# Clustered attention with two feed-forward layers: where the softmax division is done, which engine makes the one-hot comparisons, and the order of TensorE's work in a tile

## The reference

```
q_assign = argmax(normalised q . normalised centroids)      # 16 clusters
k_assign = argmax(normalised k . normalised centroids)
scores   = where(q_assign == k_assign, q k^T / 8, -1e9)
attn     = exp(scores - rowmax);  attn = attn / (rowsum + 1e-9)
out      = attn @ v
x = out as 1536 x 512
h = x @ w_in (512 x 2048);  g = P(h) / (Q(h) + 1e-6);  x = g @ w_out
h = x @ w_in2;              g = h - tanh(h);           out = g @ w_out2
```

## Time and profile before

| | |
|---|---|
| median of three runs | 822.11 us (821.48 to 824.07) |
| the profiled execution | 823.63 us, with a span of 821.8 us from the first to the last instruction |
| mean granted TensorE clock | 0.983 of full speed |
| PE busy | 791.9 us, 96% of the span |
| PEld busy | 680.3 us, 83% |
| DVE busy | 526.7 us, 64% |
| ACT busy | 501.5 us, 61% |
| POOL busy | 353.0 us, 43% |

### The profile page before, as it was taken

One profiled execution on the slowest core, in us unless ns is written; L12 is line 12 of the kernel. 1 busy time (PEld: TensorE's weight loads), 2 busy tenths in 40 slices (PEclk: granted clock), 3 DMA queues, 4 the chain that ended last, 5 costly groups with the idle time before them and its releaser, 6 DMA issues.

```text
span 821.8 us, 11654 instructions
## 1 busy us (share of the span) xinstructions
PE 791.9 (96%) x4066; PEld 680.3 (83%) x4066; DVE 526.7 (64%) x910; ACT 501.5 (61%) x954; POOL 353.0 (43%) x377
## 2 busy tenths in 40 slices
PE   5899999999999899999999999999999999999998
PEld 5789998989898787888788888888888888888886
DVE  4599889898988879999977787995311211111111
ACT  3578788888888877878776777777422222222222
POOL 5467787877877723213222222226622222222222
PEclk7699999999999999999999999999999999999999
DMA  4723323332330205200000011115100100001001
GB/s 129 188 72 76 85 73 83 85 77 72 83 74 19 68 11 154 77 0 1 1 0 1 1 51 52 52 52 170 35 1 1 51 1 1 0 9 44 1 0 52
DMA packets 39082, 41.17 MB, mean 50 GB/s; under 512 B 4720, under 2 KB 30320, under 8 KB 39024
## 3 DMA queue, kind: packets, MB, share of 16 engines
q1 hardware_dynamic: 39024, 40.42, 17.5%
HBM read 26.25 MB, written 3.15 MB: 36 GB/s over the span
## 4 chain that ended last, share of the span: by engine, by line
PE 55%; POOL 20%; DVE 13%; issue 6%; ACT 3%; SPq 2%; DMA 1%; POOLq 0%; DVEq 0%; ACTq 0%
PE y_ps L1060 27%; PE h_ps L1039 25%; POOL probs L407 9%; DVE f_bc L841 2%; DVE f_t L860 2%; DVE w_lo L815 2%; DVE f_bc L858 2%; POOL nq L416 2%; DVE f_a L854 2%; POOL v L433 1%; POOL nk L424 1%; POOL hot L441 1%; POOL x_lo L452 1%; DVE f_t L846 1%; POOL hot L442 1%
## 5 line engine op out<-in xcount | busy, mean ns | idle before, releaser
L498 POOL TENSOR_TENSOR g_lo<-f_t,g_hi 128x512 fp32r<-128x512 f32 x96 | 125.1, 1303 | 377.7 <-ACT g_hi L594 377.7
L897 DVE TENSOR_TENSOR f_t<-h_ps,f_a 128x512 f32<-128x512 f32 x48 | 33.2, 691 | 203.4 <-ACT f_a L673 203.4
L1039 PE MATMUL h_ps<-x_hi,w_hi 128*128 128x512 f32 x384 | 149.5, 389 | 1.3 <-DVE w_lo L815 1.3
L1039 PE MATMUL h_ps<-x_lo,w_hi 128*128 128x512 f32 x384 | 149.5, 389 | 0.0
L1039 PE MATMUL h_ps<-x_hi,w_lo 128*128 128x512 f32 x384 | 149.4, 389 | 0.0
L594 ACT ACTIVATE g_hi<-f_t 128x512 fp32r<-128x512 f32 x96 | 60.8, 633 | 138.8 <-PE y_ps L1060 123.4
L407 POOL TENSOR_SCALAR probs<-probs,rinv 128x768 f32<-128x768 f32 x96 | 86.3, 911 | 69.2 <-DVE rinv L782 65.9
L557 ACT ACTIVATE pt_hi<-pt_ps 128x384 fp32r<-128x384 f32 x192 | 85.3, 492 | 48.3 <-PE pt_ps L979 47.1
L788 DVE TENSOR_TENSOR pt_lo<-pt_ps,pt_hi 128x384 fp32r<-128x384 f32 x192 | 98.5, 547 | 13.8 <-ACT pt_hi L557 13.1
L775 DVE TENSOR_REDUCE nmax<-s_ps 128x1 f32<-128x768 f32 x96 | 91.0, 948 | 7.4 <-PE s_ps L966 6.5
L979 PE MATMUL pt_ps<-ident,probs 128*128 128x128 f32 x576 | 85.1, 283 | 6.7 <-POOL probs L407 5.6
(11 more groups left out here) (122 smaller groups left out, 1571.7 us busy)
## 6 DMA issues: line engine op xcount, KB each, us to landing
w_raw<-in_moe_w_in_dram SPq DMA_DIRECT2D x32, 256.0 KB, 2.9
w_raw<-in_moe_w_out_dram SPq DMA_DIRECT2D x32, 256.0 KB, 3.7
ka<-qk_b SPq DMA_DIRECT2D x32, 192.0 KB, 3.0
raw_q<-in_q_dram SPq DMA_DIRECT2D x16, 192.0 KB, 2.6
raw_k<-in_k_dram SPq DMA_DIRECT2D x16, 192.0 KB, 2.9
raw_v<-in_v_dram SPq DMA_DIRECT2D x16, 192.0 KB, 3.1
qk_b<-qa SPq DMA_DIRECT2D x16, 192.0 KB, 2.7
out_dram<-f_bc SPq DMA_DIRECT2D x12, 256.0 KB, 2.1
```

The source lines that it names most:

```text
L498: pool.tensor_tensor(g_lo[n % 2][:, :], f_t[n % 2][:, :], g_hi[n % 2][:, :].bitcast(F32), ALU.subtract).then_inc(g_lo_done, 1)
L897: dve.tensor_tensor(f_t[n % 2][:, :], h_ps[n % 4][:, :], f_a[n % 2][:, :], ALU.subtract).then_inc(g_done, 1)
L1039: last = pe.matmul(h_ps[n % 4][:, :], w[f][:, ws], x[:, cols], start=(kt == 0 and i == 0), stop=(kt == KT - 1 and i == 2))
```

## The change

The softmax division leaves the probabilities. They are transposed and multiplied with v undivided; the division is made on the finished `xf` (128 rows: two heads of 64 dimensions; 384 columns: positions). There the reciprocal belongs to a column, so the reciprocals of a half head (128 partitions x 3 columns) go by DMA to a row of 384 numbers in DRAM (`rows_out`) and back, broadcast to the 64 partitions of that head (`rows_in`); POOL multiplies (`normalise`). `row_inverse` runs once in three turns on three columns. The comparisons of `finish_hot` move from DVE to POOL in another form (subtract, then max and add, or max and multiply); the first two heads keep them on DVE (`finish_first`). On POOL `rank_hot` goes ahead of `split_k`, the two `x_low` of a pair are set apart, on ACT `copy_x` is one turn later, and on PE `score_tile` comes ahead of the units.

```diff
 # tensors
+        z_rows = nc.dram_tensor("z_rows", [HALVES, HALF], F32, kind="Internal").ap()
+        rz = [sb(attn_mem, f"rz{i}", [P, HALF]) for i in range(2)]
-        POOL_CHUNK_AT = {79: 0, 83: 1, 85: 2, 91: 3}
+        POOL_CHUNK_AT = {80: 0, 83: 1, 86: 2, 92: 3}
 # SP
+            def rows_out(hh):
+                sp.wait_ge(rinv_done, hh + 1)
+                sp.dma_start(z_rows[hh, :].rearrange("(t p) -> p t", p=P),
+                             rinv[:, HT * hh % 12:HT * hh % 12 + HT],
+                             allow_slow_non_contiguous=True).then_inc(z_out, 16)
+            def rows_in(hh):
+                s, half = divmod(hh, 2)
+                sp.wait_ge(z_out, 16 * (hh + 1))
+                if s >= 2:
+                    sp.wait_ge(norm_done, 2 * (s // 2 - 1) + half + 1)
+                sp.dma_start(rz[half][D * (s % 2):D * (s % 2) + D, :],
+                             z_rows[hh, :].partition_broadcast(D)).then_inc(rz_in[half], 16)
             for k in range(-1, TILES):
+                if k >= 0 and k % HT == 1:
+                    rows_out(k // HT)
+                if k > 0 and k % HT == 0:
+                    rows_in(k // HT - 1)
 ...
+            rows_in(HALVES - 1)
 # POOL
-            def scale_probs(m):
-                pool.wait_ge(rinv_done, m + 1)
-                hi_of(probs[m % PROBS][:, :], probs[m % PROBS][:, :], rinv[:, m % 12:m % 12 + 1]).then_inc(probs_scaled, 1)
+            def finish_hot(g):
+                pool.wait_ge(top2_done, g - FIRST + 1)
+                pool.wait_ge(prep_done, prepared(g - 1, HOT))
+                link(pool.tensor_tensor(hot_nat[:, :, :].rearrange("p a (t c) -> p (a t) c", c=C), hot[:, :, :],
+                                        top2[:, :].unsqueeze(2).broadcast_to([P, 2 * T, C]), ALU.subtract))
+                pool.tensor_scalar(hot_nat[:, 0, :], hot_nat[:, 0, :], -1.0, 1.0, ALU.max, ALU.add).then_inc(hot_done, 1)
+                pool.tensor_scalar(hot_nat[:, 1, :], hot_nat[:, 1, :], -1.0, BIG, ALU.max, ALU.mult).then_inc(hot_done, 1)
+            def normalise(pair, half):
+                pool.wait_ge(rz_in[half], 32 * (pair + 1))
+                pool.wait_ge(xf_done, 4 * pair + 2 + half + 1)
+                pool.tensor_tensor(xf[half][:, :], xf[half][:, :], rz[half][:, :], ALU.mult).then_inc(norm_done, 1)
-            for m in range(2):
-                scale_probs(m)
             for k in range(TILES):
                 if r == 0 and 3 <= (k + 18) // T < HEADS:
                     split_q((k + 18) // T)
-                if r == 1 and 3 <= (k + 17) // T < HEADS:
-                    split_k((k + 17) // T)
-                if r == 2 and 2 <= (k + 10) // T < HEADS:
-                    rank_hot((k + 10) // T)
+                if r == 1 and 2 <= (k + 11) // T < HEADS:
+                    rank_hot((k + 11) // T)
+                if r == 2 and 3 <= (k + 16) // T < HEADS:
+                    split_k((k + 16) // T)
                 if r == 3 and 1 <= (k + 3) // T < HEADS:
                     split_v((k + 3) // T)
-                if r == 5:
-                    s = (k - 11) // T
-                    if s >= 1 and s % 2 == 1:
-                        x_low(s // 2, 0)
-                        x_low(s // 2, 1)
+                if r == 4 and 2 <= (k + 8) // T < HEADS:
+                    finish_hot((k + 8) // T)
+                if r in (1, 4) and k // T >= 2 and k // T % 2 == 0:
+                    normalise(k // T // 2 - 1, r // HT)
+                if r == 5 and k // T >= 2 and k // T % 2 == 0:
+                    x_low(k // T // 2 - 1, 0)
+                if r == 0 and k // T >= 3 and k // T % 2 == 1:
+                    x_low(k // T // 2 - 1, 1)
-                if k % 2 == 0 and k + 2 < TILES:
-                    scale_probs(k + 2)
-                    scale_probs(k + 3)
             split_weights(PRELOAD)
+            normalise(LAST_PAIR, 0)
             g_low(0)
+            normalise(LAST_PAIR, 1)
             g_low(1)
 # ACT
             def copy_x(pair, half):
-                act.wait_ge(xf_done, 4 * pair + 2 + half + 1)
+                act.wait_ge(norm_done, 2 * pair + half + 1)
-                if s >= 1 and s % 2 == 1 and r in (1, 4):
-                    copy_x(s // 2, (0 if r == 1 else 1))
+                if s >= 1 and s % 2 == 1 and r in (2, 5):
+                    copy_x(s // 2, r // HT)
 # DVE
-            def row_inverse(m, count):
-                cols = slice(m % 12, m % 12 + count)
-                dve.wait_ge(exp_done, m + count)
+            def row_inverse(hh):
+                cols = slice(HT * hh % 12, HT * hh % 12 + HT)
+                dve.wait_ge(exp_done, HT * hh + HT)
+                if hh >= 4:
+                    dve.wait_ge(z_out, 16 * (hh - 3))
                 link(dve.tensor_scalar(rsum_e[:, cols], rsum[:, cols], 1e-9, None, ALU.add))
-                dve.reciprocal(rinv[:, cols], rsum_e[:, cols]).then_inc(rinv_done, count)
+                dve.reciprocal(rinv[:, cols], rsum_e[:, cols]).then_inc(rinv_done, 1)
-                if r == 3 and 2 <= (k + 9) // T < HEADS:
-                    finish_hot((k + 9) // T)
-                if k % 2 == 0 and k + 2 < TILES:
-                    row_inverse(k + 2, 2)
+                if k % HT == 0:
+                    row_inverse(k // HT)
 # PE
             def transpose_probs(k):
-                pe.wait_ge(probs_scaled, k + 1)
+                pe.wait_ge(exp_done, k + 1)
             for k in range(TILES):
                 transpose_probs(k)
+                if k + LOOK < TILES:
+                    score_tile(k + LOOK)
                 for g, u in units_at[k]:
                     if u != SIM:
                         unit(g, u)
-                if k + LOOK < TILES:
-                    score_tile(k + LOOK)
                 if k >= HT:
                     values(k)
```

More of the change, by code:

```diff
@@ L179, in clustered_attention_then_two_ffns @@
         max_done, rinv_done, pt_lo_done = sem("max_done"), sem("rinv_done"), sem("pt_lo_done")
-        sim_read, top_done, xf_done = sem("sim_read"), sem("top_done"), sem("xf_done")
-        k_lo_first, prep_copied_dve = sem("k_lo_first"), sem("prep_copied_dve")
+        z_out, rz_in, norm_done = sem("z_out"), [sem(f"rz_in{i}") for i in range(2)], sem("norm_done")
+        sim_read, top_done, top2_done, xf_done = sem("sim_read"), sem("top_done"), sem("top2_done"), sem("xf_done")
+        hot_first, k_lo_first, prep_copied_dve = sem("hot_first"), sem("k_lo_first"), sem("prep_copied_dve")
         dve_chain = sem("dve_chain")
-        probs_scaled, q_split, k_split, v_split = sem("probs_scaled"), sem("q_split"), sem("k_split"), sem("v_split")
+        q_split, k_split, v_split = sem("q_split"), sem("k_split"), sem("v_split")
         hot_ranked, hot_done = sem("hot_ranked"), sem("hot_done")
@@ L404, in link, with hi_of @@
                 pool.wait_ge(pool_chain, chain[0])
-            def hi_of(dst, src, factor=1.0):
-                return pool.tensor_scalar(dst, src, factor, 1.0, ALU.mult, ALU.mult)
+            def hi_of(dst, src):
+                return pool.tensor_scalar(dst, src, 1.0, 1.0, ALU.mult, ALU.mult)
             def split_q(g):
@@ L747, in read_top2, with finish_first @@
                 dve.wait_ge(hot_ranked, g - FIRST + 1)
-                link(dve.reduce_max(top2[:, :], hot[:, :, :], AX.X))
-            def finish_hot(g):
+                dve.reduce_max(top2[:, :], hot[:, :, :], AX.X).then_inc(top2_done, 1)
+            def finish_first(g):
                 if g > 0:
@@ L756, in finish_hot @@
                                        top2[:, T:2 * T].unsqueeze(2).broadcast_to([P, T, C]), ALU.not_equal))
-                dve.tensor_scalar(hot_nat[:, 1, :], hot_nat[:, 1, :], -BIG, None, ALU.mult).then_inc(hot_done, 1)
+                dve.tensor_scalar(hot_nat[:, 1, :], hot_nat[:, 1, :], -BIG, None, ALU.mult).then_inc(hot_first, 1)
                 dve.tensor_tensor(q_nat, hot[:, 0:T, :], top2[:, 0:T].unsqueeze(2).broadcast_to([P, T, C]),
-                                  ALU.is_equal).then_inc(hot_done, 1)
+                                  ALU.is_equal).then_inc(hot_first, 1)
             def first_hot(g):
@@ L770, in first_hot @@
                 link(dve.reduce_max(top2[:, :], hot[:, :, :], AX.X))
-                finish_hot(g)
+                finish_first(g)
             def row_max(m):
@@ L805, in _ @@
             row_max(1)
-            row_inverse(0, 1)
             row_max(2)
-            row_inverse(1, 1)
             row_max(3)
@@ L932, in unit @@
                 elif u == HOT:
-                    pe.wait_ge(hot_done, 2 * (g + 1))
+                    if g < FIRST:
+                        pe.wait_ge(hot_first, 2 * (g + 1))
+                    else:
+                        pe.wait_ge(hot_done, 2 * (g - FIRST + 1))
                     for i in range(2):
```

## The result

| | before | after |
|---|---|---|
| median of the runs | 822.61 us (821.48 to 824.07, 4 runs) | 936.12 us (934.30 to 937.77, 4 runs) |
| ratio, 95% interval | 1 | 1.1378 (1.1348 to 1.1409) |
| profiled execution, span | 823.63, 821.8 us | 936.96, 935.2 us |

The forecast was 812.2 us. The changed kernel is 113.5 us slower, far outside the range.

What follows compares the result with a forecast made beforehand. The prediction took the attention as a PE pipeline with a POOL wait in it. Terms of -8.4 (twelve heads), 0 (start), -2.5 (late attention) and +1.0 (handing over) gave -9.9 us: 812.2 us, range 806.3 to 818.9.

Steps and rivals of the forecast that it cites:

- What bounds the kernel before: Steady attention: PE is the bound and loses 0.94 us of a 16.29 us head, mostly waiting for POOL's scalings.
- What is late next is DVE: Steady heads at r = 0: DVE's second remainder still holds PE 0.23 us, taken as 0.12 a head.
- POOL beside DVE: Steady heads: POOL's operations lengthen DVE's row inverses by 0 to 1.01 us, taken as 0.3 twice; 0.12 a head reaches PE.
- The comparisons: One-hot comparisons leaving DVE: free 0.76 us of its busy time a head, leaving DVE 13.6 us in 15.35, not the bound.
- Moves of order: Steady attention: POOL's new finish_hot is hidden, scores ahead of units and extra SP issues cost 0, at most 0.2 a head.
- start: Start of the kernel: a unit moved behind PE's one-hot wait costs about what missing scalings give back: 0, from -1 to +1.
- late attention: Around 250 to 285 us: smaller POOL waits and perhaps no clock fall, -2.5 us (-1 to -3.5).
- handing over: Attention to feed-forward: two normalise on POOL slow DVE's two-input operations beside them, +1.0 us (0 to +1.6).
- `rows_out` at cost 0: SP's queue: the added issues, 2.6 us a head, cost 0 unless held up; near DMAs land after 1.8 and 4.5 us.
- The trip through DRAM holds SP: Rival, chance 0.09: rows_in waits on SP for the write; beyond 7.2 us each of 32 half heads pays; 837.8 at 8 us.
- The one-hot rows come late: Rival, chance 0.08: the 0.8 us margin before the one-hot score tile fails, PE waits 0.4 us a head: 817.0 us.
- The signs of being wrong: In the trace: rows_out landing over 7 us, SP's one-hot DMAs starting later, a head over 16, score tiles waiting for one-hot rows.

Runs made afterwards that it cites:

- e1: Changed kernel without both DMAs of the reciprocals; normalise multiplies by ones, so no division is done: 812.14 us, 0.9871 of the kernel before.
- e6: e1 with the one-hot comparisons put back on DVE in their old form: 824.33 us, 1.0017 of the kernel before.
- e7: e1 with the units again ahead of the score tile on PE: 812.53 us, 0.9884 of the kernel before.
- e14: Changed kernel writing only one column, 128 neighbouring 4-byte numbers, and reading back another tensor, without the real reciprocals: 878.74 us, one run.
- e4: Changed kernel with the 384 single numbers written 512 bytes apart and a weight row read back, without the real reciprocals: 817.04 us, 0.9931 of the kernel before.
- e2: Changed kernel with rows_in issued three turns later and four semaphores in turn for the write: 864.98 us, 1.0528 of the kernel before.
- e8: Changed kernel with reciprocals transposed on PE and written as three 512-byte runs, reading back a turn later, division whole: 815.40 us, 0.9916 of the kernel before.
- e3: Changed kernel writing the reciprocals as 128 runs of 12 bytes, so they stand in the wrong columns: 819.04 us, 0.9960 of the kernel before.
- e11: Changed kernel with the 384 single numbers written 64 bytes apart and another tensor read back, without the real reciprocals: 818.52 us, one run.
- e15: Changed kernel with the 384 single numbers written 8 bytes apart and another tensor read back, without the real reciprocals: 821.49 us, one run.
- e12: Changed kernel with the 384 single numbers written 16 bytes apart and another tensor read back, without the real reciprocals: 818.07 us, one run.
- e9: Changed kernel with 12-byte runs, division whole by stepped reading, rows_in a turn later, last trips behind weight loads: 816.13 us, 0.9917 of the kernel before.
- e10: Kernel before with only the reciprocals' trip through DRAM and back added, its result unused: 906.84 us, 1.1011 of the kernel before.
- e13: Changed kernel with only the reading changed: another tensor is read back, without the real reciprocals; the neighbouring writes stay: 894.28 us, one run.

## Why the prediction was wrong, step by step

**What bounds the kernel before: right.** e1 takes the scaling off PE's path and the head falls from 16.29 to 15.61 us; 15.59 was forecast.

**"What is late next is DVE": right.** In e1 PE's only wait for an engine's result from 50 to 240 us has the size of the earlier trace rows:

```profile
PEld pt_ps L1010 <- DVE pt_lo L820: 1.2, 6, 0.2
```

No wait on POOL is left before the transposes. DVE's work for a head is 0.8879 x 15.61 = 13.9 us, 13.6 forecast.

**"POOL beside DVE", 0 to 1.01 us for each row inverse: right in kind, smaller in e1.** The prediction took 0.3 us more for each. In e1 the row sum has a mean of 0.26 us against 0.16 at its shortest, so 0.1 more; the longest is 0.60. The trace of e6 agrees with the Trainium skill here (GPSIMD Engine Reference, Key points), which names contention for the shared SBUF interfaces; how long it holds, the row at 112.48 shows.

**The comparisons: mis-sized.** The prediction took their 0.76 us a head as DVE's slack, and put the gain down to the scaling. e6 shows that the slack isn't where they stood: without moving them the division gains nothing. The mean hid it: a busy share of 0.89 says nothing of the one turn in which two chains meet. That the sum came out is luck in this part, since the change makes both moves and the prediction only had to be right for the two together.

**Moves of order, `finish_hot`, start, late attention, handing over: right within what can be told.** e7 moves 0.4 us; the start is +0.2 (0 forecast), but the first steady SIM lies anywhere from 47.8 to 51.1 us in the runs without slow writes, so that small terms of the start are not told; behind the last SIM e1 has -2.6 (-1.5 forecast), and the clock from 250 to 260 us no longer falls (1.00, 0.88 in the earlier trace rows). That sum was -9.9; e1 measures 812.14 - 822.69 = -10.6.

**The step that failed: `rows_out` at cost 0.** The landing was taken from the two nearest rows, 1.8 and 4.5 us, as if landing time were a matter of size and of class. Neither row has many tiny elements side by side, and that is what costs: about 10.2 us here. The place was right, SP standing in `rows_in`. A head of 15.6 us leaves each round 15.6 / 2 - 1.15 = 6.65 us for the write (7.2 in the rival); the excess of 10.2 - 6.65 = 3.55 us is paid twice a head, 24 x 3.55 = 85 us in the twelve heads, and measured it is 12 x (22.64 - 15.61) = 84.4.

This is the sum of the rounds turned about, not a second proof, and as a threshold it fails elsewhere: e14, where the landings on the chain are 6.8 to 8.2 us, should by the rival's formula lose some 32 x (7.6 - 7.2) = 13 us and loses 62 against e4, and e2 loses 53 against e1 with SP hardly held.

The rival "The trip through DRAM holds SP" by its own formula would give 32 x (10.2 - 7.2) - 9.9 = +86 at this landing; it had 0.09, because both near rows lay low, although no row bounded the operation from above. Most of the 27 us that are missing there is the handing over, which it didn't price: the same wait holds weight chunks, and PE stands for 24.5.

**What the rival had not either**: other DMAs land late beside such a write. The one-hot rows land after 6.2 us in the change and 4.4 in e2, where SP hardly waits. The rival "The one-hot rows come late" had PE wait 0.4 us a head; it is 59.1 / 12 = 4.9 here, and not by the order of scores and units, which costs nothing in e7, but mostly by the landing.

The Trainium skill (DMA: Bandwidth & Descriptors, Specifications) says that a transfer needs at least 512 bytes for the full rate, and that below it a read-modify-write is done. The direction agrees, e8's 512-byte runs among the good ones. The size rule alone doesn't fit: the 12-byte runs (2.6 us) and the spaced singles (1.8 us) lie as far below it and are quick.

**The signs of being wrong** came, but for one: `rows_out` landed over 7 us, the head was over 16, score tiles waited for one-hot rows. The one-hot DMAs starting later in the head came only in part, by 0 to 3.6 us.

**Left open.** Why neighbours of 4 bytes are slow is not shown. That two elements are written into the same 8 bytes can't be the whole of it: e3's runs do that as often as e14's numbers do, and are quick. By which way reading the row back adds 42 us is open too, and so is whether the one-hot rows only stand behind the write. e11 to e15 are single runs; the differences on which their readings rest are 40 us and more, those among e11, e12 and e15 are not relied on beyond the landing times.

## What to carry to other kernels

An operation that no row of the trace shows has no upper bound from its nearest rows: measure it by itself, or keep its price out of the likely case, above all where a queue waits for its landing. Lay a column out as a row in DRAM with runs (here 12 or 512 bytes), never as neighbouring single numbers, and place the loads that others need ahead of such a trip. Reading later helps where the landing is long (e2: 71 us), and gained nothing in the heads where it is 2.6 us (e9). And when an engine is freed of work, ask which turn had no room, not what its mean share is.

## What the runs showed of the hardware

- 384 numbers of 4 bytes written from 128 partitions to neighbouring DRAM addresses land after 7 to 12 us (chains of the change, e10 and e13; 8.3 is e2's median), with 8 bytes between starts 3.9, 16 bytes 2.8, 64 bytes 2.2, 512 bytes 1.8; 128 runs of 12 bytes 2.6.
- 128 neighbouring numbers of 4 bytes land after 6.8 to 8.2 us (e14, three landings on its chain).
- Beside such a write 16 KB transfers of the same queue land after 4.4 to 6.2 us instead of 1.8; six of them issued over 3.5 us landed within 1.3 us, just behind the write.
- Each element of such a write is a packet: 8192 fewer of them for 32 x 256 fewer elements (e3 against the change).
- A DVE operation of 0.16 us on SBUF (128x3) lasted 0.97 us and ended with a POOL operation of 1.01 us.
- A step of 12 bytes in one operand costs POOL 1.13 instead of 1.01 us for 128x384.
